# One row per partition for the block inputs of an mLSTM scan, tanh gates, and expert weights in 512 KB pieces

## The reference

```python
for t in range(S):                       # B, H, S, D = 4, 8, 768, 40
    m_new = np.maximum(f_gate[:, :, t] + m, i_gate[:, :, t])
    f_stab = np.exp(f_gate[:, :, t] + m - m_new)
    i_stab = np.exp(i_gate[:, :, t] - m_new)
    C = f_stab * C + i_stab * outer(vt, kt)
    n = f_stab * n + i_stab * kt
    denom = np.maximum(np.abs(sum(n * qt)), 1.0)
    y[:, :, t] = 1.0 / (1.0 + np.exp(-o_gate[:, :, t])) * (C @ qt) / denom
# x = y as (3072, 320)
logits = x @ phi                         # softmax over tokens: d; over slots: c
slot_out[e] = np.maximum((d.T @ x)[e] @ w1[e], 0.0) @ w2[e]    # 8 experts, F = 1024
x = c @ slot_out
out = ((x @ w_a) * (x @ w_b)) @ w_out    # 3072 x 320 -> 1536 -> 320
```

## Time and profile before

| | us |
|---|---|
| median of 3 runs | 292.0 |
| lowest and highest | 290.67 and 293.09 |
| the profiled execution | 291.69 |
| its span, first to last instruction | 289.9 |

### The profile page before, as it was taken

The page is one execution under the profiler, slowest core; times in us unless marked ns, Lnnn a source line. Parts: engine busy times, 40 slices in busy tenths (PEclk is TensorE's granted clock), DMA queues, the critical chain, the costliest instruction groups (busy, mean ns, idle before and its releaser), DMA issues.

```text
span 289.9 us, 7961 instructions
## 1 busy us (share of the span) xinstructions
PE 252.0 (87%) x3288; PEld 208.9 (72%) x3288; DVE 183.2 (63%) x463; ACT 89.6 (31%) x147; POOL 62.0 (21%) x92
## 2 busy tenths in 40 slices
PE   0558698855999599999899999999799999999996
PEld 0547687845899599998748826556656668999995
DVE  6963577852787468788718714355986867555550
ACT  3683511120322122232415004343800003444441
POOL 9502142311325132517211401421000000000000
PEclk9999999995999899999999999999979999999999
DMA  7927867689759975640499999970000000322222
GB/s 235 364 56 240 229 185 198 181 361 262 208 157 367 272 204 142 192 144 5 172 443 410 425 409 451 406 282 0 2 0 0 0 2 0 115 90 90 83 79 90
DMA packets 20131, 54.73 MB, mean 189 GB/s; under 512 B 3744, under 2 KB 14144, under 8 KB 18432
## 3 DMA queue, kind: packets, MB, share of 16 engines
q1 hardware_dynamic: 20096, 54.23, 54.2%
HBM read 49.99 MB, written 4.23 MB: 187 GB/s over the span
## 4 chain that ended last, share of the span: by engine, by line
PE 57%; SPq 15%; DVE 12%; DMA 10%; issue 3%; ACT 2%; DVEq 0%
PE ps L936 50%; DMA attn<-kk 8%; SPq L380 6%; SPq L386 4%; PE ps L1153 3%; DVE attn L703 2%; SPq L375 2%; PE ps L1027 2%; ACT xTreg L545 1%; SPq L404 1%; DMA scratch_G<-xTreg 1%; PE ps L1159 1%; SPq L398 1%; DMA xTreg<-ig 1%; DVE attn L716 1%
## 5 line engine op out<-in xcount | busy, mean ns | idle before, releaser
L936 PE MATMUL ps<-attn 128*64 128x41 f32 (+3 forms) x2016 | 91.6, 252 | 17.2 <-DMA attn<-kk 9.6
L936 PEld LDWEIGHTS ps<-attn 128*64 128x64 f32 (+1 forms) x2016 | 85.8, 139 | 24.5 <-DMA attn<-kk 10.2
L491 POOL TENSOR_TENSOR attn<-attn 128x160 f32<-128x160 f32 x48 | 21.2, 462 | 84.0 <-issue 53.4
L703 DVE SCALAR_TENSOR_TENSOR attn<-attn,small,ps 128x41 f32<-128x41 f32 x176 | 30.9, 248 | 4.4 <-PE ps L936 4.4
L545 ACT COPY xTreg<-ps 128x512 f32<-128x512 f32 x24 | 13.6, 593 | 61.6 <-PE ps L1027 61.6
L936 PE MATMUL ps<-woreg,tlow 128*128 128x320 f32 x96 | 28.2, 456 | 2.5 <-DVE tlow L886 2.5
L936 PE MATMUL ps<-Whr,Phr 128*128 128x320 f32 x96 | 30.0, 313 | 0.0
L936 PE MATMUL ps<-Whr,Plr 128*128 128x320 f32 x96 | 29.7, 309 | 0.0
L936 PE MATMUL ps<-Wlr,Phr 128*128 128x320 f32 x96 | 29.6, 309 | 0.0
L686 DVE TENSOR_TENSOR attn<-ps,attn 128x512 f32<-128x512 f32 x24 | 16.5, 688 | 18.6 <-issue 12.1
L936 PEld LDWEIGHTS ps<-woreg,tlow 128*128 128x128 f32 x96 | 18.3, 198 | 12.1 <-DVE tlow L886 4.8
(11 more groups left out here) (157 smaller groups left out, 335.9 us busy)
## 6 DMA issues: line engine op xcount, KB each, us to landing
attn<-kk SPq DMA_DIRECT2D x24, 416.0 KB, 4.2
front<-w SPq DMA_DIRECT2D x2, 2560.0 KB, 10.3
tail<-w SPq DMA_DIRECT2D x2, 2560.0 KB, 12.1
xTreg<-w SPq DMA_DIRECT2D x4, 1280.0 KB, 12.9
attn<-v SPq DMA_DIRECT2D x48, 82.0 KB, 3.1
xreg<-og SPq DMA_DIRECT2D x4, 960.0 KB, 7.0
attn<-qT SPq DMA_DIRECT2D x48, 80.0 KB
xreg<-w SPq DMA_DIRECT2D x3, 1280.0 KB, 11.0
```

The costliest lines, as they stand in the source:

```text
L491: last = g.tensor_tensor(ksb[n % 2][:, c, 0:HU * D].rearrange("r (h e) -> r h e", h=HU), knb[n % 3][:, c], last_col[:, c].unsqueeze(2).to_ ...
L703: last = v.scalar_tensor_tensor(out=C[:, cc + 1, p], in0=C[:, cc, p], scalar=dcy[:, 2 * u + p, cc:cc + 1], in1=pUv[:, p, c, 0:VW], op0=ALU ...
L936: return t_.matmul(o_, l_, r_, start=start, stop=stop)
```

## The change

The inputs of a block become one array `blk_in[u, blk, a]` with a contiguous row of 1672 elements (6688 B) for each of 64 partitions and each half a. The upper half's row is q, v, k feature-major, k token-major; the lower half's is k, k token-major, v, q, placed 840 columns later, so that the columns which must be zero in one half are those that the other half fills beyond the common part. `qb`, `vb`, `kb`, `knb` become views into four buffers `in_b`. A block is two transfers, on one semaphore, sent once all five counters of block n - 4 are there. 24 of 64 rows of q are padding. To make room `Wb` moves into `Ed`.

Blocks 0 to 2 are sent at the start, each when its own buffer is zeroed, then og of batch 0; og 1 follows behind the exponent rows of unit 1, og 2 and og 3 behind blocks 6 and 12. w1 groups 0 and 1 become ten transfers of 512 KB, one behind each of blocks 4 to 15 except 6 and 12; groups 2 and 3 are ten transfers too.

The gate is tanh(x / 2) / 2 + 1/2, as a Tanh and a Copy with scale and bias, per unit (960 elements a partition): units 0 and 1 ahead of the scan, unit n // 3 + 1 behind Exp(n) for n = 4, 7, ..., 19. The parts of G are written with even chunks first, so that the exponent rows of one parity are read in runs of 768 B instead of 128 B.

```diff
             return a - n
-        qb = [view(take(4 * CB * L), 4 * CB * L).rearrange("r (p h t) -> r p h t", p=2, h=2) for _ in range(NQ)]
-
         KF, KT = 2 * CB * L, 2 * HU * D
-        kkb = [view(take(KF + KT), KF + KT) for _ in range(3)]
-        kb = [x[:, 0:KF].rearrange("r (p t) -> r p t", p=2) for x in kkb]
-        knb = [x[:, KF:KF + KT].rearrange("r (c h e) -> r c h e", c=2, h=HU) for x in kkb]
-        VB = 2 * HU * VW + 8
-        vb = [view(take(2 * VB), 2 * VB).rearrange("r (a n) -> r a n", a=2) for _ in range(NQ)]
+        QF, VF = 2 * CB * L, 2 * HU * VW
+        HALF, OTHER = QF + VF + KF + KT, QF + VF
+        in_b = [view(take(HALF + OTHER), HALF + OTHER) for _ in range(NQ)]
+
+        def two(x, c0, pairs):
+
+            return bass.AP(tensor=x.tensor, offset=x.offset + c0, ap=[list(x.ap[0])] + pairs)
+
+        qb = [two(x, 0, [[CB * L, 2], [HALF + VF, 2], [1, CB * L]]) for x in in_b]
+        vb = [two(x, QF, [[VF + KF + KT, 2], [1, VF + 8]]) for x in in_b]
+        kb = [x[:, OTHER:OTHER + KF].rearrange("r (p t) -> r p t", p=2) for x in in_b]
+        knb = [x[:, OTHER + KF:HALF].rearrange("r (c h e) -> r c h e", c=2, h=HU) for x in in_b]
         LE = [view(take(S // 2), S // 2).bitcast(BF16) for _ in range(2)]
         RE = [view(take(HU * S // 4), HU * S // 4).bitcast(BF16).rearrange("r (h c t) -> r h c t", h=HU, c=NCP)
               for _ in range(2)]
-        Wb = [view(take(512), 512).rearrange("r (c h t) -> r c h t", c=2, h=HU) for _ in range(2)]
+        Wb = [Ed[:, 8 * i:8 * i + 8].rearrange("r (c h) t -> r c h t", c=2) for i in range(2)]
         Eb = [view(take(512), 512) for _ in range(2)]
...
@@ -338,6 +342,14 @@
                             cs[0:R_MASK + R_B, C_R + L * h:C_R + L * h + L].unsqueeze(1).to_broadcast([R_MASK + R_B, NCP, L]))
             return last
 
+        def by_par(x):
+
+            return x.rearrange("r (c a t) -> r c a t", a=2, t=L)
+
+        def halves(k):
+
+            return PT[:, k, 0:S].rearrange("r (a c t) -> r c a t", a=2, t=L)
+
         def turn_ps(m):
 
             return psT if m < NB - 6 else [psT, psE[0], psE[1]][(m - NB) % 3]
...
-                t0, tn = blk * CB * L, CB * L
-                if n >= 3:
-                    sp.wait_ge(s_ps, n - 2)
-                    sp.wait_ge(ks_sb, n - 2)
-                sp.dma_start(kkb[n % 3], kk[u, blk]).then_inc(ld_k[n % 3], 16)
                 if n >= NQ:
-                    sp.wait_ge(x_ps, n - NQ + 1)
-                for hp in range(2):
-                    rows = slice(64 * hp, 64 * hp + D)
-                    sp.dma_start(qb[n % NQ][rows, :, hp, :], qT[u, hp, :, :, t0:t0 + tn]).then_inc(ld_q[n % NQ], 16)
-                if n >= NQ:
-                    sp.wait_ge(u_ps, n - NQ + 1)
-                    sp.wait_ge(y_ps, n - NQ + 1)
-                for par in range(2):
-
-                    sp.dma_start(vb[n % NQ][64 * par:64 * par + 64, par, 0:2 * HU * VW],
-                                 v1[u, 64 * par:64 * par + 64, blk, :]).then_inc(ld_v[n % NQ], 16)
+                    done = n - NQ + 1
+                    sp.wait_ge(s_ps, done)
+                    sp.wait_ge(ks_sb, done)
+                    sp.wait_ge(u_ps, done)
+                    sp.wait_ge(y_ps, done)
+                    sp.wait_ge(x_ps, done)
+                else:
+                    sp.wait_ge(zeroed, n + 1)
+                for a in range(2):
+                    sp.dma_start(in_b[n % NQ][64 * a:64 * a + 64, OTHER * a:OTHER * a + HALF], blk_in[u, blk, a]).then_inc(ld_b[n % NQ], 16)
...
-                    src = scr_G[:, u * HU:(u + 1) * HU].rearrange("k h (c a t) -> k h c a t", a=2, t=L)
-                    sp.dma_start(RE[r][rows], src[:, :, :, par, :]).then_inc(ld_exp[r], 16)
-
-            for b in range(B - 1):
-                sp.dma_start(xtok[:, b], og[b]).then_inc(ld_og[b], 16)
-            sp.wait_ge(zeroed, 4)
-            load_block(0)
+                    src = scr_G[:, u * HU:(u + 1) * HU].rearrange("k h (a s) -> k h a s", a=2)
+                    sp.dma_start(RE[r][rows].rearrange("r h c t -> r h (c t)"), src[:, :, par, :]).then_inc(ld_exp[r], 16)
+
+            for n in range(3):
+                load_block(n)
+            sp.dma_start(xtok[:, 0], og[0]).then_inc(ld_og[0], 16)
 
             sp.wait_ge(parts_b, 1)
             sp.dma_start(scr_b, PT[:, :, S:2 * S]).then_inc(b_out, 16)
             sp.wait_ge(parts_G, 1)
             sp.dma_start(scr_G.rearrange("k h s -> h k s"), PT[:, :, 0:S]).then_inc(G_out, 16)
             load_exponents(0)
-            load_block(1)
-            sp.dma_start(xtok[:, B - 1], og[B - 1]).then_inc(ld_og[B - 1], 16)
-            load_block(2)
             load_block(3)
             load_exponents(1)
+            sp.dma_start(xtok[:, 1], og[1]).then_inc(ld_og[1], 16)
             sp.dma_start(phis, phi).then_inc(ld_phi, 16)
             for n in range(4, NB):
                 load_block(n)
                 if n % NBLK == 1 and n // NBLK + 1 < NU:
                     load_exponents(n // NBLK + 1)
-                if n in (8, 14):
-                    sp.dma_start(w1s[n // 12], w1[n // 12]).then_inc(ld_w1p[n // 12], 16)
+                if n in (6, 12):
+                    sp.dma_start(xtok[:, n // 6 + 1], og[n // 6 + 1]).then_inc(ld_og[n // 6 + 1], 16)
+                elif 4 <= n < 16:
+                    j = n - 4 - (n > 6) - (n > 12)
+                    cols = slice(j % 5 * F, j % 5 * F + F)
+                    sp.dma_start(w1s[j // 5][:, cols], w1[j // 5, :, cols]).then_inc(ld_w1p[j // 5], 16)
 
             sp.wait_ge(y_ps, NB)
...
-                sp.dma_start(w1s[i], w1[i]).then_inc(ld_w1p[i], 16)
+                for j in range(5):
+                    cols = slice(j * F, j * F + F)
+                    sp.dma_start(w1s[i][:, cols], w1[i, :, cols]).then_inc(ld_w1p[i], 16)
             sp.wait_ge(one["logits_ps"], 2)
...
-                g.memset(vb[r][:].rearrange("r a n -> r (a n)"), 0.0)
-                g.memset(qb[r][:].rearrange("r p h t -> r (p h t)"), 0.0).then_inc(zeroed, 1)
+                g.memset(in_b[r][:, 0:OTHER], 0.0)
+                g.memset(in_b[r][:, HALF:HALF + OTHER], 0.0).then_inc(zeroed, 1)
             for r in range(2):
                 g.memset(ksb[r][:, :, HU * D:KSW], 0.0)
                 g.memset(Cb[r][:, 0], 0.0).then_inc(C_zero, 1)
...
-                left = g.tensor_tensor([GR, PT[:, 2]][k][:, 0:S], [GB, GR][k][:, 0:S], PT[:, k, 0:S], ALU.subtract)
-                left.then_inc([R_done, parts_G][k], 1)
+            pool.wait_ge(cut_done, 1)
+            g.tensor_tensor(by_par(GR[:, 0:S]), by_par(GB[:, 0:S]), halves(0), ALU.subtract).then_inc(R_done, 1)
+            pool.wait_ge(cut_done, 2)
+            g.tensor_tensor(halves(2), by_par(GR[:, 0:S]), halves(1), ALU.subtract).then_inc(parts_G, 1)
             pool.wait_ge(parts_G, 1)
 
             def gate(u):
...
                 for p in range(2):
                     last = g.tensor_tensor(x[:, p], x[:, p], dnb[u % 2][:, 1, p].unsqueeze(2).to_broadcast([128, NC, D]), ALU.mult)
                 last.then_inc(gate_done, 1)
 
...
 
-            def sigmoid(b):
-                act.wait_ge(ld_og[b], 16)
-                s.activation(xtok[:, b], xtok[:, b], ACT.Sigmoid).then_inc(sig_done, 1)
-
+            def sigmoid(u):
+
+                act.wait_ge(ld_og[u // 2], 16)
+                x = xtok[:, u // 2, :, 80 * (u % 2):80 * (u % 2) + 80]
+                s.activation(x, x, ACT.Tanh, scale=0.5).then_inc(tanh_done, 1)
+                act.wait_ge(tanh_done, u + 1)
+                s.activation(x, x, ACT.Copy, scale=0.5, bias=0.5).then_inc(sig_done, 1)
 
             act.wait_ge(G_done, 1)
-            s.copy(PT[:, 0, 0:S], GB[:, 0:S]).then_inc(cut_done, 1)
+            s.copy(halves(0), by_par(GB[:, 0:S])).then_inc(cut_done, 1)
             s.activation(eG, GB[:, 0:S], ACT.Exp).then_inc(eG_done, 1)
             act.wait_ge(R_done, 1)
-            s.copy(PT[:, 1, 0:S], GR[:, 0:S]).then_inc(cut_done, 1)
-            for b in range(B - 1):
-                sigmoid(b)
+            s.copy(halves(1), by_par(GR[:, 0:S])).then_inc(cut_done, 1)
+            for u in range(2):
+                sigmoid(u)
 
             def xT_evac(m):
...
-                if n == 2:
-                    sigmoid(B - 1)
                 act.wait_ge(e_ps, n + 1)
                 if n >= 2:
                     act.wait_ge(w_sb, n - 1)
                     act.wait_ge(ks_sb, n - 1)
                 s.activation(Eb[n % 2], psE[n % 2][:], ACT.Exp).then_inc(e_sb, 1)
+                if n >= 4 and n % NBLK == 1 and n // NBLK + 1 < NU:
+                    sigmoid(n // NBLK + 1)
...
-    kk = np.concatenate([kf, kn.reshape(NU, NBLK, 128, 2 * HU * D)], -1)
+        x = x.reshape(NU, 2, D, 2, NBLK, CB * L).transpose(0, 4, 1, 2, 3, 5)
+        return np.pad(x, ((0, 0), (0, 0), (0, 0), (0, 64 - D), (0, 0), (0, 0))).reshape(NU, NBLK, 2, 64, 2 * CB * L)
+
+    qf, kf = feature_major(q), feature_major(k)
```

(4 more changed lines are left out.)

34 lines of the change are left out of this document (12 added, 22 removed).

## The result

The changed kernel takes 306.2 us (median of 4 runs, 304.89 to 307.97) against 291.34 for the kernel before in the same session. The ratio is 1.052, with a 95% interval of 1.048 to 1.057: slower by 15 us, where 16 us of gain were forecast. The profiled execution has a span of 303.5 us.

What follows compares the result with a forecast made beforehand. It took PE to be stalled by loads queued behind w1 in the one queue, plus early DMA waits. Gains 12.96 + 3.3 + 0.2 = 16.5 us gave 275.2 from the profiled 291.69, so 275.5 for the median; range 272.0 to 281.0.

Steps and rivals of the forecast that it cites:

- the supply: DMA queue in the scan: 350 GB/s or more estimated from row lengths, against 330 demanded while w1 pieces run.
- Each transfer bears its own fixed time: Rival: half-height or 512 KB transfers do not overlap; below 247 GB/s over blocks 3 to 15 it decides; chance 0.03.
- 3.5 of slack: Block loads in the scan: about 3.5 us of queue delay assumed to be absorbed before it costs time.
- The 3.3 us of the first six blocks: Early DMA waits of PE go through fewer issues and blocks 0 to 2 loaded early: 3.3 us gained, bounds 0 and 3.3.
- about 22: Sign expected in the profile: block 0 to block 6 in about 22 us.
- 0.2 taken: Exponent rows read in 768 B runs may land earlier: 0.2 us gained, bounds 0 and 0.6.
- The 12.96 us: Two scan stalls behind 2560 KB pieces of w1 go when w1 is cut: 12.96 us gained, bounds 9.0 and 12.96.
- The gates: Tanh and Copy per unit on ACT, 1.0 us each, 2.1 a pair, hidden in ACT's waits: cost 0.
- the rival of table loads: Rival: tanh needs its own table, two more loads of 1.28 us a pair, 9.6 us in all, so 285; chance 0.04.
- The wait for block n - 4: Block loads wait for all five counters of block n-4; cost 0, covered by about 10 us of slack.
- the ten pieces of the tail: Behind the scan, w1 of experts 4 to 7 in ten pieces instead of two transfers: cost 0.
- The clock rival: Rival: low PE clock behind the scan costs 2.2 us; if the shift in time spares it, 273.3; chance 0.12.

Runs made afterwards that it cites:

- e1: Changed kernel with both halves of a block loaded into the same columns by one 128-partition transfer, output not the reference's; 276.65 us, ratio 0.949.
- e5: Changed kernel with half 0 sent to the even and half 1 to the odd partitions, data wrong for the matmuls; 274.32 us, ratio 0.943.
- e4: Changed kernel with block rows 6912 B apart in memory instead of 6688, each starting at a multiple of 256 B; 305.94 us.
- e7: Kernel before with one edit: w1 in the scan as ten 512 KB pieces behind blocks 5 to 14; 287.37 us, ratio 0.986.
- e10: Kernel before with only the gates changed to Tanh and Copy per unit; 291.35 us, ratio 1.000.

## Why the prediction was wrong

**The step that failed is the supply.** "New rows are 6.7 KB and 4 KB, nearest to the last row and longer, so I take 350 or more as an estimate." The rate was read off row lengths. The row it was taken from (348 GB/s) was of full-height transfers, and so were all the large ones in the trace of before. The new ones are half-height, and in that form the queue gives 222 GB/s (60 to 80 us), w1's pieces between them slowed as well. e1 and e5 move the same rows of 6688 B at 357 once a transfer covers all 128 partitions or every second of them; e4 shows that their place in memory does not matter. Joining k to q and v turned the one large full-height transfer of a block, kk, into half-height ones too.

**The rival nearest to what happened was in the text, with a chance of 0.03.** "Each transfer bears its own fixed time" put the tipping point at 247 GB/s for blocks 3 to 15. With 222 its own sum gives 19.3 / 0.222 = 87 us for 58, 29 less 3.5 of slack, 25 us of stalls, which makes 301 us; measured are 306.2. By the marks, block 6 to block 16 takes 119.37 - 50.57 = 68.8 us against 42.3 undisturbed (three units and a step), 26.5 lost, and 13.0 in the kernel before. The 3.3 us of the first six blocks did not come either. The price was about right and the mechanism wrong: not a time per transfer (e5 has as many transfers, of the same size), but the half of the partitions that a transfer stays in. The sentence "today's transfers of 80 to 416 KB already run at 302 at full share" was the wrong evidence against it, since over half of the bytes of a block in it were kk at full height, and about half of v's short packets escape; their slowest tenth, 125 ns or more for 56, was there to be seen in the packets.

**Right, once the rate is there.** e1 (276.65) and e5 (274.32) are the change as forecast, with the rate that the forecast had assumed: 275.5. By the marks of e5, block 0 to 6 takes 45.59 - 24.20 = 21.4 us ("about 22"), 4.0 less than before where 3.3 was taken. Block 0 comes 0.8 earlier (0.2 taken), and blocks 6 to 23 take 72.1 instead of 84.4: 12.3 gained where 12.96 was taken. The sum, 17.1, stands beside 16.5. The parts are less sure than the sum: block 0 comes at 25.33 in e1, which has the same start, so its 0.8 us are scatter, and e1 as a whole gains 14.6.

**The 12.96 us do not belong to the pieces alone.** The forecast gave all of it to cutting w1 and nothing to the fewer issues. By e7 the pieces alone gain 4, since SP then needs 13.6 us or more a unit, 1.2 of it for the exponent rows. With two issues a block and the full rate, in e5, blocks 6 to 23 gain the 12.3 above. The total held in e5, its division did not.

**The gates, right.** Tanh and Copy take 1.00 us each, as taken, with a single table load in the whole program, and e10 measures no difference. So the rival of table loads is out, and the trace agrees with the statement of the Trainium skill, "ScalarE: Activation LUTs", section "Table sets: the hidden batching unit", that exp and tanh share a set, which no row of before could show.

**The wait for block n - 4 and the ten pieces of the tail cost nothing**: in e5 PE waits for no load in the scan, and from the clock's fall at the z products on the changed kernel runs as the old one did, 76.53 us of PE in the chain for 76.52.

**The clock rival did not come true in this kernel, but it exists.** It was priced at 2.2 us; where it comes it gives back 1.2 (last section).

## What to carry to other kernels

Before you join small transfers into large ones, look at which partitions the result covers: a transfer to the lower or upper 64 partitions alone moved at 222 to 234 GB/s here, one over all 128, or over every second of them, at 357 to 406, and full-height pieces between half-height loads were slowed to half as well. Sending a third of zeros to stay full height was faster than leaving them out. Take the rate of a planned transfer from a row of the same partitions, not of the same length; DMA share at 9 with a low GB/s beside it on the page is how the slow form shows. And an edit that adds issues to a queue (pieces) is to be priced with all that the queue issues in the same period, each at its own time (0.37 us for kk, 0.84 for one of q in e7).
